# Denominators of a Mish inverted in pairs, and weight subtractions divided between two engines

## The reference

```python
q_pool = q.reshape(B, H, S // 2, 2, D).mean(axis=3)       # B 2, H 8, S 1152, D 64
attn = softmax(q_pool @ k.T / sqrt(D)) @ v                # rows x of 1152 tokens x 512
# layer 0, d_ff 2048 (Mish)
h = x @ w_in
g = h * tanh(log1p(exp(min(h, 20))))
x = g @ w_out
# layer 1 (ELU)
h = x @ w_in2
g = where(h > 0, h, exp(min(h, 0)) - 1)
out = g @ w_out2
```

## Time and profile before

| | |
|---|---|
| median of 3 runs | 662.42 us |
| profiled execution, own time | 662.09 us |
| its span in the trace | 660.2 us |
| TensorE busy | 651.6 us, 99% |
| VectorE busy | 408.3 us, 62% |
| ScalarE busy | 393.6 us, 60% |
| GpSimd busy | 400.9 us, 61% |
| granted TensorE clock | 1.0 of full speed |

### The profile page before, as it was taken

One profiled execution on the slowest core, in us unless ns is written; L12 is line 12 of the kernel. 1 busy time (PEld: TensorE's weight loads), 2 busy tenths in 40 slices (PEclk: granted clock), 3 DMA queues, 4 the chain that ended last, 5 costly groups with the idle time before them and its releaser, 6 DMA issues.

```text
span 660.2 us, 12323 instructions
## 1 busy us (share of the span) xinstructions
PE 651.6 (99%) x4042; PEld 641.8 (97%) x4042; DVE 408.3 (62%) x645; ACT 393.6 (60%) x733; POOL 400.9 (61%) x352
## 2 busy tenths in 40 slices
PE   8899999999999999999999999999999999999998
PEld 7799999999999999999999999999999999999997
DVE  7787878888888853778788767874433232223222
ACT  5689889889889888567465447764433222222220
POOL 5577797988888684889745455986344422222221
PEclk9999999999999999999999999999999999999999
DMA  6656767676566511212200001222212010001001
GB/s 206 167 157 186 196 167 196 179 216 169 166 174 182 154 44 42 83 52 77 65 0 0 0 16 49 81 65 64 65 65 65 17 48 0 0 0 48 1 1 49
DMA packets 35856, 57.93 MB, mean 88 GB/s; under 512 B 7568, under 2 KB 13024, under 8 KB 35808
## 3 DMA queue, kind: packets, MB, share of 16 engines
q1 hardware_dynamic: 35488, 57.02, 30.7%
q10 hardware_dynamic: 320, 0.30, 0.2%
HBM read 33.29 MB, written 2.40 MB: 54 GB/s over the span
## 4 chain that ended last, share of the span: by engine, by line
PE 95%; DVE 1%; DMA 1%; ACT 1%; issue 0%; POOL 0%; ACTq 0%; DVEq 0%; POOLq 0%
PE py L584 10%; PE pH L569 10%; PE pH L568 10%; PE py L583 10%; PE py L582 10%; PE pH L567 10%; PE pm L486 6%; PE po L515 6%; PE ps L500 6%; PE ps L501 6%; PE po L516 6%; PE po L517 6%; DMA q<-q_sum 1%; DVE pl L855 0%; DMA q_raw<-qT 0%
## 5 line engine op out<-in xcount | busy, mean ns | idle before, releaser
L1099 POOL TENSOR_TENSOR gl<-fg,gh 128x384 fp32r<-128x384 f32 x96 | 97.5, 1015 | 161.8 <-ACT gh L761 158.4
L835 DVE TENSOR_REDUCE part_max<-pm 128x1 f32<-128x384 f32 x225 | 118.5, 549 | 33.2 <-PE pm L486 30.8
L932 DVE RECIPROCAL fr<-fd 128x384 f32<-128x384 f32 x48 | 122.4, 2551 | 18.0 <-ACT fd L746 16.8
L568 PE MATMUL pH<-xl,win_h 128*128 (+1 forms) x384 | 128.3, 334 | 0.0
L569 PE MATMUL pH<-xh,win_l 128*128 (+1 forms) x384 | 128.3, 334 | 0.0
L567 PE MATMUL pH<-xh,win_h 128*128 (+1 forms) x384 | 128.3, 334 | 0.0
L584 PE MATMUL py<-gh,wout_l 128*128 128x384 f32 x384 | 128.3, 334 | 0.0
L582 PE MATMUL py<-gh,wout_h 128*128 128x384 f32 x384 | 128.3, 334 | 0.0
L583 PE MATMUL py<-gl,wout_h 128*128 128x384 f32 x384 | 128.3, 334 | 0.0
L1034 POOL TENSOR_TENSOR pl<-p,ph 128x576 fp32r<-128x576 f32 x64 | 91.4, 1433 | 41.8 <-ACT p L673 41.7
L667 ACT ACTIVATE ph<-ps 128x576 fp32r<-128x576 f32 x144 | 93.9, 652 | 28.6 <-PE ps L501 26.7
(11 more groups left out here) (77 smaller groups left out, 1266.1 us busy)
## 6 DMA issues: line engine op xcount, KB each, us to landing
kh<-k_hi SPq DMA_DIRECT2D x60, 144.0 KB, 3.3
w_raw<-w_in SPq DMA_DIRECT2D x32, 256.0 KB, 2.7
w_raw<-w_out SPq DMA_DIRECT2D x32, 256.0 KB, 2.6
q_raw<-qT SPq DMA_DIRECT2D x16, 288.0 KB, 3.1
k_pack<-kP SPq DMA_DIRECT2D x16, 288.0 KB, 3.3
v_raw<-v SPq DMA_DIRECT2D x16, 288.0 KB, 3.5
kl<-k_pack SPq DMA_DIRECT2D x32, 144.0 KB, 2.4
q<-q SPq DMA_DIRECT2D x16, 144.0 KB, 2.5
```

The source lines that it names most:

```text
L568: pe.matmul(out, hi, xb, start=False, stop=False)
L932: dve.reciprocal(fr[:, b, :], fd[:, b, :]).then_inc(r_ready, 1)
```

## The change

A product of two denominators is inverted once. The 384 columns of `fd` are taken as two halves a and b of 192 (`HT`). GpSimd multiplies them, `fp` = a * b. VectorE takes the reciprocal of the 192 columns of `fp` into `fi`, and multiplies `fi`, repeated twice, with `fd` with its halves exchanged: b/(ab) = 1/a and a/(ab) = 1/b, into `fr`. On GpSimd, `finish_mish` and `split_g` of a unit now stand in the step of the next unit, with the new `multiply_d` between them, and the last unit's stand behind layer 0. `low_w` in layer 0 is divided as in layer 1: VectorE for even units, behind `divide`, and GpSimd for odd ones, behind `split_g` of the unit before.

```diff
+    HT = TT // 2
...
+            fp = sf("fp", [P, 2, HT])
+            fi = sf("fi", [P, 2, HT])
...
             def divide(f, u):
 
                 b = f % 2
+                dve.wait_ge(prod_ready, u + 1)
+                dve.reciprocal(fi[:, b, :], fp[:, b, :]).then_inc(prod_inv, 1)
+                dve.wait_ge(prod_inv, u + 1)
                 wait(dve, mish_ready, u - 1)
-                dve.wait_ge(d_ready, u + 1)
-                dve.reciprocal(fr[:, b, :], fd[:, b, :]).then_inc(r_ready, 1)
+                dve.tensor_tensor(halves(fr[:, b, :]), halves(fd[:, b, :])[:, ::-1, :],
+                                  fi[:, b, :].unsqueeze(1).to_broadcast([P, 2, HT]), ALU.mult).then_inc(r_ready, 1)
...
-                if f % 2 == 0 and layer:
+                if f % 2 == 0:
                     low_w(dve, layer, t, i, f)
...
+            def multiply_d(f, u):
+
+                b = f % 2
+                pool.wait_ge(d_ready, u + 1)
+                wait(pool, prod_inv, u - 1)
+                pool.tensor_tensor(fp[:, b, :], fd[:, b, 0:HT], fd[:, b, HT:TT], ALU.mult).then_inc(prod_ready, 1)
...
             def unit_step(layer, t, f, u, i):
                 if layer == 0:
-                    finish_mish(f, u)
-                    low_w(pool, layer, t, i, f)
-                    split_g(f, u)
+                    first = isinstance(u, int) and u == 0
+                    if not first:
+                        finish_mish((f + 3) % 4, u - 1)
+                    multiply_d(f, u)
+                    if not first:
+                        split_g((f + 3) % 4, u - 1)
                 else:
                     split_g(f, u)
-                if f % 2 == 1 and layer:
+                if f % 2 == 1:
                     low_w(pool, layer, t, i, f)
...
+                if layer == 0:
+                    finish_mish(NF - 1, UNITS - 1)
+                    split_g(NF - 1, UNITS - 1)
```

More of the change, by code:

```diff
@@ L156, in build @@
         t_ready, a_ready, sq_ready, d_ready = sem("t_ready"), sem("a_ready"), sem("sq_ready"), sem("d_ready")
-        r_ready, mish_ready = sem("r_ready"), sem("mish_ready")
+        prod_ready, prod_inv, r_ready, mish_ready = sem("prod_ready"), sem("prod_inv"), sem("r_ready"), sem("mish_ready")
         e_ready, e_capped, elu_ready = sem("e_ready"), sem("e_capped"), sem("elu_ready")
```

## The result

The changed kernel takes 666.88 us, median of four runs (666.19 to 667.73), against 662.25 us for the kernel before (661.82 to 662.79) with the same number of runs. The ratio is 1.0068, 95% interval 1.0056 to 1.0081. The forecast was 668.6 us in a range of 662.6 to 675.

What follows compares the result with a forecast made beforehand. TensorE was taken to bound the kernel, with a unit due every 4.16 us, so the change could only eat reserve. Waits of 3.0 + 0.8 + 2.7 = 6.5 us on 662.09 us gave 668.6 us, range 662.6 to 675.

Steps and rivals of the forecast that it cites:

- product on GpSimd: Layer 0, each unit: GpSimd's product for 192 columns takes 0.59 us, with bounds 0.5 and 0.8.
- multiplication, free: Layer 0: VectorE's new 384-column multiplication, with nothing in its way, takes 0.555 us, bounds 0.46 and 0.8.
- multiplication in odd units, from its start: Tiles 0 and 2: multiplication waits behind GpSimd's weight subtraction, running 1.44 to 2.83 in the unit's cycle, not to 2.00.
- fg in even units: Tiles 0 and 2: GpSimd's fg, ready at 2.10, gets through only behind VectorE's weight subtraction, ending at 3.47.
- r of unit 15 ends: End of tile 0: unit 15's multiplication result is done at 330.6, after pairs of 8.5 us and two additions.
- held in tile 0: Tile 0: TensorE waits 3.0 us, spread over small waits, as pairs take 8.5 us where 8.32 are due.
- before g2 of unit 16: Into tile 1: low_y stands behind unit 17's multiplication, so y is freed late; TensorE waits 0.8 us more.
- before g2 of unit 48: Into layer 1: late unit 47 and the following chain delay the copies of y; TensorE waits 2.7 us more.
- the price of a turn: Two-SBUF-input VectorE operations and GpSimd operations take turns; the second pays its whole length but about 0.14 us.
- The last term: The wait into layer 1, before g2 of unit 48: 2.7 us of the 6.5 us sum.
- no turns: Rival, chance 0.14: no blocking, a pair takes 7.6 us; only unit 4 is tight; 662.1, at most 662.6 us.
- Only the tiles are late: Rival, chance 0.14: turns cost, but the multiplication is short and tile 2's y is freed in time; 663.1 to 664.5 us.

Runs made afterwards that it cites:

- The kernel with the supposed order: Changed kernel with ScalarE's weight copy of layer 1's first tile moved behind gh in every unit; 670.13 us, ratio 1.0120.

## Why the prediction was right, and what in it was wrong

The direction, the mechanism and the places of the waits were right. By its steps:

| step | predicted | measured |
|---|---|---|
| reciprocal of 192 columns | 1.35 us | 1.353 us |
| product on GpSimd | 0.59 us | 0.601 us |
| multiplication, free | 0.555 us | 0.558 us |
| multiplication in odd units, from its start | 1.39 us | 1.33 to 1.50 us |
| fg in even units | 1.37 us | 1.40 us |
| r of unit 15 ends | 330.6 | 330.90 |
| held in tile 0 | 3.0 us | 2.9 us |
| before g2 of unit 16 | 0.8 us | 0.8 us |
| before g2 of unit 48 | 2.7 us | 1.0 us |

The first eight hold, with the waits at the places where they were put, because the rows of layer 1 already held the price of a turn, and because the sum was made per unit against the 4.16 us that are due, not on busy shares: VectorE's share fell and GpSimd's share stood at 63%, and neither tells of this loss. One figure among the prediction's signs doesn't fit its own working: "about 1.0 us in odd units" for the multiplication, where its cycle has 1.39 us (1.44 to 2.83) and the trace 1.33 to 1.50. By the rule of the Trainium skill ("SBUF — State Buffer", section "Who interferes with whom") a multiplication on VectorE with two SBUF inputs contends with a GpSimd operation that reads SBUF, and one with a single SBUF input, outside the two-port modes, does not; the trace agrees, with 1050 ns against 554 ns for the same work. That section says the shared ports are an exclusive lock, and says of VectorE's two-port modes that whoever issues first keeps them for its whole instruction and the other is fully blocked. Here, with a multiplication of two inputs, 0.13 to 0.15 us of the second one's length are already spent when its turn comes, as in the earlier trace rows.

The last term was mis-sized: it makes up 1.7 of the 1.9 us by which the sum of the waits, 6.5 us, lies above the 4.6 measured. The step that failed is "gh 48 at 468.5, weight copy at 469.1 ... VectorE's weight subtraction comes behind GpSimd's gl 48 and ends at 470.2". In the code, ScalarE's weight copy of a unit in layer 1 stands ahead of exp and gh, not behind them; I had taken over the order of layer 0. The trace of the kernel before shows this order too, in lines that the earlier trace rows leaves out. The copy at 456.64 there is that of unit 49. The copy of unit 48 ran at 454.78, ahead of exp 49 and gh 48, and VectorE's subtraction at 455.79, before gh 48 was done and so ahead of gl 48.

```profile
454.78 0.62 ACT L677 ACTIVATE wout_h<-w_raw 128x512 fp32r<-128x512 f32 x1
455.48 0.49 ACT L752 ACTIVATE fe<-pH 128x384 f32<-128x384 f32 x1
455.91 0.53 ACT L761 ACTIVATE gh<-fg 128x384 fp32r<-128x384 f32 x1
...
455.79 0.68 DVE L266 TENSOR_TENSOR wout_l<-w_raw,wout_h 128x512 fp32r<-128x512 f32 x1
```

The timeline of ScalarE and then VectorE in the changed kernel:

```profile
465.90 1.28 ACT L755 ACT_TABLE_LOAD   x1
467.20 0.49 ACT L755 ACTIVATE fe<-pH 128x384 f32<-128x384 f32 x1
467.58 0.62 ACT L680 ACTIVATE wout_h<-w_raw 128x512 fp32r<-128x512 f32 x1
468.11 0.49 ACT L755 ACTIVATE fe<-pH 128x384 f32<-128x384 f32 x1
468.71 0.53 ACT L764 ACTIVATE gh<-fg 128x384 fp32r<-128x384 f32 x1
...
471.69 1.62 ACT L799 ACTIVATE xh<-py 128x384 fp32r<-128x384 f32 x4
...
468.59 0.68 DVE L269 TENSOR_TENSOR wout_l<-w_raw,wout_h 128x512 fp32r<-128x512 f32 x1
...
472.20 1.95 DVE L955 TENSOR_TENSOR xl<-py,xh 128x384 fp32r<-128x384 f32 x4 [0.97 <-ACT xh L799]
```

The weight copy comes at 467.58, VectorE's subtraction at 468.59, ahead of GpSimd's gl and at its free 0.68 us. So the copies of y start at 471.69 and not at 473.1. The kernel with the supposed order shows the supposed time: the copies start at 473.02, where 473.1 was worked out, and the wait is 2.8 us.

Of the rivals, "no turns" gave 662.1 to 662.6 us, and that is the time of the kernel with the inverse in PSUM, 662.39. "Only the tiles are late" fell because TensorE was held before unit 48 too, and its range of 663.1 to 664.5 us ends 2.4 us below the measured time. No kernel here beats the kernel before: in the two layers it already leaves TensorE no wait, and the best of the others only get back to it.

## What to carry to other kernels

Before work is moved off a busy engine, look at where its operands lie: a VectorE operation with two SBUF inputs beside a busy GpSimd can cost the rest of GpSimd's operation as well, here 1.3 to 1.5 us in place of 0.56 (and GpSimd's 1.40 in place of 1.02), and an operand in a PSUM bank that is free at that time avoided it. In a pipeline whose bound is another engine, compare the longest cycle through the helpers with the time due per unit, and the reserve at the first units and at tile boundaries; shares of busy time don't show either. Take the order of instructions at a boundary from the code of that stage, not from its neighbour.

## What was not expected of the hardware

The wait of 2.7 us before unit 48 in the kernel with the late weight copy cost more than itself. These are the stretches around it (length, busy PE, PEld, DVE, ACT, POOL, granted clock, DMA share, GB/s), and two matmuls behind the wait:

```profile
471.00:474.00 3.00, 0.65 (x4) 0.33 (x2) 1.54 (x4) 2.71 (x7) 2.11 (x2) 1.00 0.32 87
474.00:478.00 4.00, 3.86 (x13) 3.86 (x14) 3.73 (x9) 2.57 (x6) 1.50 (x3) 0.57 0.43 100
478.00:482.00 4.00, 4.00 (x25) 4.00 (x24) 0.22 (x1) 1.45 (x4) 2.58 (x3) 1.00 0.30 96
...
474.97 0.52 PE L585 MATMUL py<-gh,wout_h 128*128 128x384 f32 x1
475.29 0.52 PE L586 MATMUL py<-gl,wout_h 128*128 128x384 f32 x1
```

TensorE starts a matmul every 0.32 us in place of 0.17 from 474.65 to 477.85, and the granted clock over the four microseconds is 0.57: half speed, 1.2 GHz, for most of them. Before, TensorE had done next to nothing for 2.7 us. Ten matmuls 0.15 us late are 1.5 us, which is the difference between the 3.3 us measured and the wait's own growth of 1.8. In the traces, the changed kernel's wait of 0.9 us at the same place, and one of 1.5 us in the kernel with the paired reciprocal alone, left the clock at 1.00. The second may not always do so: all four executions of the kernel with the late weight copy have a mean clock of 0.997, and so has one execution of the kernel with the paired reciprocal alone, 676.10 us against 675.10 in the traced one at 1.00. No trace shows where that one lost its clock.
